# Strided sparse attention into a rational MLP on one core: an order drawn from plays with shared DMA queues and instruction lines, small matmuls in pieces, and the last 512 tokens in two chunks

## What is computed

```python
rel = pos[:, None] - pos[None, :]
mask_local = (rel >= 0) & (rel < 32)                                   # heads 0 to 3
mask_strided = (rel >= 0) & (pos[None, :] % 32 == pos[:, None] % 32)   # heads 4 to 7
attn = softmax(where(mask, q @ k.T / 8, -1e9)) @ v
x = attn.transpose(0, 2, 1, 3).reshape(4608, 512)
h = x @ w_in                                                           # 512 -> 2048
P = a[0] + a[1] * h + a[2] * h**2 + a[3] * h**3
Q = 1 + |b[0]| * |h| + |b[1]| * h**2
out = (P / (Q + 1e-6)) @ w_out                                         # 2048 -> 512
```

## Time and profile before

| | us |
|---|---|
| median of 3 runs | 437.22 |
| lowest, highest | 433.15, 437.31 |
| the profiled execution's own time | 436.66 |
| its span, first to last instruction | 434.8 |

### The profile page before, as it was taken

One profiled execution on the slowest core, in us unless ns is written; L12 is line 12 of the kernel. 1 busy time (PEld: TensorE's weight loads), 2 busy tenths in 40 slices (PEclk: granted clock), 3 DMA queues, 4 the chain that ended last, 5 costly groups with the idle time before them and its releaser, 6 DMA issues.

```text
span 434.8 us, 10010 instructions
## 1 busy us (share of the span) xinstructions
PE 339.6 (78%) x4494; PEld 170.3 (39%) x4540; DVE 322.3 (74%) x237; ACT 313.5 (72%) x332; POOL 110.0 (25%) x122
## 2 busy tenths in 40 slices
PE   1636975768997987488787989699899989958437
PEld 1426334434453443234433545254445434423212
DVE  5232198796989587568859879988989789897760
ACT  3211557296978796298749988888889999979732
POOL 6950391670009238063225320000000000000000
PEclk9999996696998999699969999699999999969959
DMA  9999999994559999999949994121121101101102
GB/s 192 173 205 134 163 174 141 150 170 65 115 154 88 148 172 178 148 144 174 129 116 126 175 115 105 24 54 73 30 51 51 50 1 48 50 0 48 48 0 96
DMA packets 140466, 46.52 MB, mean 107 GB/s; under 512 B 112376, under 2 KB 135160, under 8 KB 140280
## 3 DMA queue, kind: packets, MB, share of 16 engines
q0 software_dynamic: 77024, 17.19, 48.5%
q1 hardware_dynamic: 63112, 28.56, 35.9%
q10 hardware_dynamic: 288, 0.14, 0.1%
HBM read 36.87 MB, written 17.69 MB: 125 GB/s over the span
## 4 chain that ended last, share of the span: by engine, by line
PE 41%; ACT 26%; DVE 13%; DMA 11%; issue 8%; SPq 1%
PE ps L898 15%; PE ps L958 14%; ACT u L932 8%; ACT u L927 7%; ACT z L914 4%; ACT h L903 4%; PE ps L852 4%; DMA ptS<-pS 4%; DMA coef<-in_moe_b_dram 3%; DMA ptL<-pL 2%; PE ps L726 2%; DVE h L944 2%; DVE u L923 2%; DMA XT<-xl 2%; DVE z L941 2%
## 5 line engine op out<-in xcount | busy, mean ns | idle before, releaser
L958 PE MATMUL ps<-Wout,h 128*128 128x512 bf16 x557 | 142.3, 395 | 25.7 <-DVE h L944 19.8
L898 PE MATMUL ps<-XT,Win 128*128 128x512 bf16 x549 | 144.5, 398 | 12.3 <-issue 6.4
L903 ACT ACTIVATE h<-ps 128x512 bf16<-128x512 f32 x144 | 80.7, 620 | 38.1 <-PE ps L898 37.3
L958 PEld LDWEIGHTS ps<-Wout,h 128*128 128x128 bf16 x576 | 56.2, 101 | 95.4 <-DVE h L944 21.8
L898 PEld LDWEIGHTS ps<-XT,Win 128*128 128x128 bf16 x576 | 54.8, 102 | 78.6 <-issue 15.5
L927 ACT ACTIVATE u<-u,consts 128x2048 bf16<-128x2048 bf16 x36 | 70.4, 2005 | 3.7 <-DVE u L923 3.6
L932 ACT ACTIVATE u<-u 128x2048 bf16<-128x2048 bf16 x36 | 67.0, 1914 | 0.0
L914 ACT ACTIVATE z<-h 128x2048 bf16<-128x2048 bf16 x32 | 60.1, 1941 | 0.1
L476 POOL DMA_DIRECT2D lq<-in_q_dram x14 | 31.2, 2230 | 81.3 <-DMA skT<-sk 81.3
L944 DVE TENSOR_TENSOR h<-z,u 128x4096 bf16<-128x4096 bf16 x18 | 41.2, 2290 | 2.6 <-ACT u L932 2.2
L592 POOL DMA_DIRECT2D vN<-in_v_dram x32 | 37.9, 2283 | 18.3 <-PE ps L783 16.9
(11 more groups left out here) (76 smaller groups left out, 291.0 us busy)
## 6 DMA issues: line engine op xcount, KB each, us to landing
out_dram<-os SPq DMA_DIRECT2D x36, 256.0 KB, 2.4
vN<-in_v_dram POOLq DMA_DIRECT2D x32, 72.0 KB, 12.9
vS<-in_v_dram POOLq DMA_DIRECT2D x32, 72.0 KB, 10.8
Win<-in_moe_w_in_dram POOLq DMA_DIRECT2D x8, 256.0 KB, 15.0
Wout<-in_moe_w_out_dram POOLq DMA_DIRECT2D x4, 512.0 KB, 7.1
lq<-in_q_dram POOLq DMA_DIRECT2D x14, 144.0 KB, 6.6
lk<-in_k_dram POOLq DMA_DIRECT2D x14, 144.0 KB, 7.6
sq<-in_q_dram POOLq DMA_DIRECT2D x7, 288.0 KB, 9.2
```

The costliest lines, as they stand in the source:

```text
L898: r = e.matmul(bank(ph, 0, CH), Win[:, kk, f * 128:(f + 1) * 128], XT[:, kk, c * CH % XC:c * CH % XC + CH], start=(kk == 0), stop=(kk == N ...
L903: P.op("act", lambda e, f=f, ph=ph, h=h: e.activation(h.t[:, f % G, :], bank(ph, 0, CH), AF.Copy), 0.597, ky, r=[ph], w=[h], occ=0.494)
L958: r = e.matmul(bank(po, 0, Fout), groups[g].t[:, j, m * 128:(m + 1) * 128], Wout[:, kk, :], start=(kk == 0), stop=(kk == NF - 1))
```

## The change

The planner keeps its list scheduling (now `_draw`) and gains three things: a count of PE's instructions in lines of 256, with 3.5 us from the end of one line to the arrival of the one after the next; a second simulation, `_play`, that runs a finished order with two DMA queues which slow each other down; and a loop that draws an order, plays it, feeds the landing times of the play back (averaged with the earlier ones) and keeps the order with the shortest play of twelve. Each PE operation carries its number of instructions `ni` (8 unless given).

```diff
+LINE, FETCH = 256, 3.5
+DRAWS = 12
...
+    def _fetch(self, st, t, o, commit):
+        cnt, land = st[0], st[1]
+        step = o.dur / o.ni
+        left = o.ni
+        while left:
+            line, at = divmod(cnt, LINE)
+            if at == 0 and line >= 2:
+                t = max(t, land[line])
+            n = min(left, LINE - at)
+            t += n * step
+            cnt += n
+            left -= n
+            if cnt % LINE == 0:
+                nx = max(t, land.get(line + 1, 0.0)) + FETCH
...
+    def _draw(self, lag):
...
+                    if e == "pe" and o.ni > 20 and s <= t0 + 1e-9:
+                        late = self._fetch(line, s, o, False) - s - o.dur
+                        if late > 0.3:
+                            s += late
...
+                if lag is None:
...
+                else:
+                    o.fin = t + lag[o]
+            elif e == "pe":
+                o.fin = self._fetch(line, t, o, True)
+                free[e] = o.fin
...
+    def _play(self):
...
+        def rate(k):
+            if not (que[0] and que[1]):
+                return 1.0
+            return 0.38 if k else 0.46 if que[1][0].dma[2:] else 0.27
...
+    def schedule(self):
+        for o in self.ops:
+            o.deps0 = dict(o.deps)
+        lag, best = None, None
+        for n in range(DRAWS):
+            self._draw(lag)
...
+            span = self._play()
+            if best is None or span < best[0]:
+                best = (span, keep)
+            new = {o: o.fin - o.start for o in self.ops if o.dma is not None}
+            lag = new if lag is None else {o: 0.5 * (x + lag[o]) for o, x in new.items()}
```

```diff
-        def lscore(e):
+        def lscore(e, g):
             r = None
-            for g in range(3):
...
+        for g in range(3):
+            P.op("pe", lambda e, g=g: lscore(e, g), 16 * 0.012, key, r=[lqt, lkt], m=[SL], ni=32)
...
-        P.op("pe", sscore, 128 * 0.009, ky, r=[T_c, sqt, skt], m=[SS])
+        for i in range(4):
+            P.op("pe", lambda e, i=i: sscore(e, i), 32 * 0.0095, ky, r=[T_c, sqt, skt], m=[SS], ni=64)
...
-            P.op("pe", sav, 64 * 0.010, key, r=[ptS, vS], w=[A])
+            for j in range(2):
+                P.op("pe", lambda e, sav=sav, j=j: sav(e, j), 32 * 0.0145, key, r=[ptS, vS],
+                     ni=64, **(dict(m=[A]) if j else dict(w=[A])))
```

```diff
+    for src, t, T in ((q, sq0, T_s0[0]), (k, sk0, T_s0[1])):
+        for b4 in range(4):
+            P.op("sp", lambda e, src=src, t=t, b4=b4: e.dma_start(
+                view0(t, 72, 2048)[:, 512 * b4:512 * b4 + 512],
+                bass.AP(tensor=src.tensor, offset=src.offset + HL * S * D + 512 * b4, ap=[[2048, 72], [1, 512]])),
+                0.45, -15e5 + b4, w=[T[b4]], dma=(0.45, 1.9))
```

```diff
-    def mlp(c, key):
+    def mlp(t0, n, gf, key):
...
+        fb = 512 // n
+        W = gf * n
+        part = W / 4096
...
+                    for j in range(fb):
+                        for kk in range(NK1):
+                            r = e.matmul(bank(ph, j * n, n), Win[:, kk, (f + j) * 128:(f + j + 1) * 128],
+                                         XT[:, kk, t0 % XC:t0 % XC + n], start=(kk == 0), stop=(kk == NK1 - 1))
...
+    todo = [(CH * c, CH, G) for c in range(NT // CH - 1)]
+    at = NT - CH
+    for n, gf in [(256, 8), (256, 8)]:
+        todo.append((at, n, gf))
+        at += n
```

More of the change, by code:

```diff
@@ L96, in op @@
         o.pre = [d for d in dict.fromkeys(pre)]
+        o.ni = ni
         for t in r:
@@ L127, in _place @@
         return best
-    def schedule(self):
+    def _fetch(self, st, t, o, commit):
[12 more added lines that the diff above has]
+                nx = max(t, land.get(line + 1, 0.0)) + FETCH
+                if commit:
+                    land[line + 2] = nx
+                elif line + 2 not in land:
+                    land = dict(land)
+                    land[line + 2] = nx
+        if commit:
+            st[0] = cnt
+        return t
+    def _draw(self, lag):
         E = self.ENG
         for o in self.ops:
-            o.then = []
+            o.then, o.users = [], []
+            o.deps = dict(o.deps0)
+            for b in o.banks:
+                b.left = 0
         for o in self.ops:
@@ L147, in schedule @@
         dmafree = {}
+        line = [0, {0: 0.0, 1: 0.0}]
         for o in self.ops:
@@ L805, in attention @@
         t0 = b * S
-        war = []
-        for c in range(t0 // CH, (t0 + S - 1) // CH + 1):
-            war += up_of.get(c - XC // CH, [])
+        war = [o for x, n, ops in up_of if x + XC < t0 + S and t0 < x + n + XC for o in ops]
         for t in T_xl[b]:
@@ L921, in mlp, with pair @@
-            dv(lambda e, z=z, u=u: e.tensor_scalar(u.t[:, :, :], z.t[:, :, :], b1_ap, b0_ap, op0=Alu.mult, op1=Alu.add),
+                dur = 0.2 + (dur - 0.2) * part
+                return P.op("dve", fn, dur, ky + dk * part, occ=dur - 0.08, **kw)
+            def pair(fn, dur, dk, **kw):
+                half = W // 2
+                dur = 0.165 + (dur - 0.165) * part
+                return [P.op("act", lambda e, i=i: fn(e, slice(half * i, half * i + half)), dur, ky + dk * part, occ=dur - 0.1,
+                             **({k: [x[i]] if k == "after" else x for k, x in kw.items()})) for i in range(2)]
@@ L949, in mlp @@
+            dv(lambda e, zf=zf: e.tensor_scalar(zf, zf, a_ap[0], None, op0=Alu.add), 1.28, 13, m=[z])
+            dv(lambda e, zf=zf, uf=uf, hf=hf: e.tensor_tensor(hf, zf, uf, op=Alu.mult), 2.28, 14, r=[z, u], m=[h])
+            groups.append((h, hf.rearrange("p (g c) -> p g c", c=n)))
+        ky = key + 46 * n / 512
         ends = []
[L950 removed]
+        for m in range(n // 128):
             po = Banks(1)
[L952 to L964 removed]
@@ new lines, in mlp, with mm @@
+            for f0 in range(0, NF, 4):
+                h, hv = groups[f0 // gf]
+                def mm(e, m=m, f0=f0, po=po, hv=hv):
+                    r = None
+                    for kk in range(f0, f0 + 4):
+                        r = e.matmul(bank(po, 0, Fout), hv[:, kk % gf, m * 128:(m + 1) * 128], Wout[:, kk, :],
+                                     start=(kk == 0), stop=(kk == NF - 1))
+                    return r
+                kw = dict(m=[po]) if f0 else dict(w=[po])
+                if f0 == 0 and m >= OPEN:
+                    kw["after"] = ends[m - OPEN:m - OPEN + 1]
+                last = P.op("pe", mm, 0.864, ky + m * 7.6 + f0 * 0.475, r=[h, T_wout[f0 // 8]], **kw)
```

307 lines of the change are left out of this document (172 added, 135 removed).

## The result

| | before | after |
|---|---|---|
| median in the runs beside each other, us | 436.68 | 421.35 |
| lowest, highest | 433.15, 437.31 | 420.62, 423.06 |
| ratio, 95% interval | | 0.967 [0.961, 0.973] |
| the profiled execution, its span | 436.66, 434.8 | 421.98, 420.2 |

Faster by 3.3%; forecast were 418 us, from 402 to 435. The total came near, and the three terms behind it did not. I cut each profiled span at two instructions of VectorE (DVE) that every version has: the first operation of its first MLP group after the absolute value (L921, now L1079), and the same operation of the sixteenth group, the last that has 4096 columns after the change.

A forecast was written before the change was run, and what follows sets the result against it. No engine was taken as full; DVE and ACT wait for a stage in front, partly PE's instruction-fetch stalls. 436.7 - 11 (middle) - 2 (start) - 6 (tail) = 417.7, so 418 us, range 402 to 435.

The forecast's parts named there:

- The tail, forecast -6: Last 512 tokens as two chunks of 256: shorter final matmuls -5.5, DVE waits -2.2, added operations +1.3 and +0.6 us.
- half should go: -2.2: Tail: DVE's waits of 2.20 and 2.21 us for ACT halve, as the pair of ACT passes is half as long.
- the 1.3 forecast: Tail: cost of 16 more DVE operations at 80 ns each, 1.3 us, within 0 to 3.5.
- ACT's 0.6 us: Tail: cost of 12 more ACT passes, taken as 0.6 us within 0 to 2.3.
- The middle, forecast -11: From 60 to 270 us: line planning removes most of PE's 14.9 us of stalls before small attention matmuls, 11 us gained.
- The reading of the stalls as line ends: PE stalls before small attention matmuls come when a line of some 256 instructions ends before the next is fetched; 14.9 us.
- the second rival: Fetch stalls move to the next boundary without shrinking; only start and tail gain, 429 us; chance 0.23.
- I take 0 beyond the fetch term: Middle: truer DMA landing times and the redrawn order bring 0 us besides fewer fetch stalls; bounds 22 us either way.
- The start, forecast -2: Start: loads in quarters and sqT copies set before the coef operation gain 2 us, within 1.3 to 3.4, or 0.
- The coef wait: Start: DVE waits 3.35 us for coef before copying sqT; the planner can set the copy first.
- Banks: Rival: waiting pieces hold PSUM banks, so up-projections wait for ACT's copies; 28 to 30 us lost, 446 us; chance 0.15.
- The order gaining more: Rival: the better drawn order speeds 60 to 270 us by 22, with start -3 and tail -6: 406 us; chance 0.17.

The follow-up runs named there:

- e1: The changed kernel with its last 512 tokens as one chunk of 512 again; 430.2 us, ratio 0.983 to the kernel before.
- e6: The kernel before with only the last 512 tokens split into two chunks of 256; 425.9 us, ratio 0.978 to the kernel before.
- e2: The changed kernel with the planner's fetch time set from 3.5 us to 0, pieces and plays kept; 422.0 us, ratio 0.965 to the kernel before.
- e4: The changed kernel with the start of before (two whole loads, transposes and copies by column block); 411.7 us, ratio 0.941 to the kernel before.
- e7: The changed kernel, same planned order, its eight start copies writing two neighbouring elements one after the other; 416.1 us, ratio 0.950 to the kernel before.
- e12: e7 with the planner also told, as in e9, that a q or k load holds SP 2.8 us; 416.7 us, ratio 0.956 to the kernel before.
- e11: e7 with the spacing of the chunks' keys at 33.1 for 33.0, altering only the order drawn; 421.4 us, ratio 0.968 to the kernel before.
- e13: e4 with the planner also told, as in e9, that a load holds SP 2.8 us; 411.6 us, ratio 0.942 to the kernel before.
- e9: The changed kernel with the planner told that each transposing q or k load holds SP 2.8 us, not 1.25; 420.2 us, ratio 0.964 to the kernel before.

## Why the forecast was right in its sum and wrong in its terms

**The tail, forecast -6, measured -9.2 (at its place 9.9 in e1 and 9.3 in e6).** The mechanism held, and one term was mis-sized. The drain after the last DVE operation went from 14.4 us (420.35 to 434.8) to 8.6 (411.57 to 420.2), -5.8 for -5.5; its matmuls, of which 15 are recorded, began at the lower level of the clock and were in the right range, against 11.24 us in the earlier trace rows. PE alone (busy, granted clock, DMA share, GB/s):

```profile
411.60:414.40 2.80, 2.60 (x6) 0.54 0.00 0
414.40:417.00 2.60, 2.50 (x9) 0.84 0.00 0
```

The step that failed is "half should go: -2.2". On DVE the stretch fell from 49.1 to 45.7 us, -3.4 where -2.2 + 1.3 were forecast. The waits for ACT there, 0.67 + 2.20 + 2.21 = 5.1 us before, are down to the 0.66 at 403.30. Four half groups give the planner two to interleave, so one runs where the other waits: two of them take 15.2 us together (387.43 to 402.63), 7.6 each, while the last, alone, takes 8.27 (403.30 to 411.57); half of a full group's 14.7 would be 7.34. So all of the waits but 0.66 went, -4.4, and the smaller operations cost 45.7 - 0.66 - 3 x 14.7 = 1.0 us for the 1.3 forecast. ACT's 0.6 us were not seen on the path.

**The middle, forecast -11, measured -5.7 (good to some 5 us).** The reading of the stalls as line ends held: the trace shows them again at regular distances, 0.9 to 4.2 us long. Two steps failed. First, "the planner now counts instructions in lines of 256 ... and postpones a piece that would stall". Counted in matmul and load records the longer stalls come some 253 apart, but some matmul records are missing: after's trace has all 4604 weight loads and only 4548 of as many matmuls. Second, that what PE waits is what the time loses: of 7.2 us of stalls gone, some came back as the wait for ptS, and e2 has 5.2 us more of them and the same time. That the model does not shorten the program was the second rival's core ("each saved stall is paid at the next boundary"), although the stalls did fall. "I take 0 beyond the fetch term" failed too: from e6 to e4, which adds line model, plays, pieces and the planner's new durations to the tail with the start of before, the time falls by 14 us. The first three were taken back only with the new start, where it does not show, and the durations never.

The sentence of the Trainium skill that the prediction weighed ("Runtime: NRT & Kernel Launch", "Instruction fetch mechanics": crossing a block is mostly hidden) would have left hardly a stall before or after; the 8 us stall of e2 speaks against that where small matmuls run in a row. For what the line model is worth to the time, nothing that e2 can tell, its 0 was nevertheless nearer than my 11.

**The start, forecast -2, measured +0.4 at the first group.** The coef wait of the earlier trace rows did go: the copies of sqT come first. The step that failed is the price of the edit as SP issues and PE waits alone: the changed copies were not priced at all. Eight copies at 1.4 to 1.6 us for 0.48 cost 3.7 and 4.9 us at the first group (e7, e12), more than the 1.3 to 3.4 us that were to be won. With the copies mended the quarters do bring what was forecast: the first group starts at 51.28, 51.45 and 51.91 us in e7, e11 and e12, and at 54.02 and 53.17 in e4 and e13, which have the old start. That e4 is 9.6 us faster all the same comes from the order drawn with the old start, in the middle; that the quarters as such cost it is not shown.

**The rivals.** Banks: PE's waits at L1053 (was L898) for ACT's copies of `h` are 0.6 us, so it did not come. The order gaining more is where e4 comes nearer, at 411.7 for its 406. So 418 came out near 421.35 by luck in part: the tail gave 3 us more than forecast, and a start that lost and a middle that gave half took away 7.7.

Of what was to show it: the drain is under 8 us, 6.0 from DVE's end (411.57) to the end of the last copy (417.58, row below), and the order of the copies is as said; the small stalls, at 7.7 us, miss the 6; DVE is at 83.6% from 60 to 330 us, just over the 83.

```profile
416.98 0.60 ACT L1112 ACTIVATE os<-ps 128x512 f32<-128x512 f32 x1 [0.27 <-PE ps L1103]
```

## What to carry to other kernels

Price an edit by every instruction whose access pattern it alters, also when the counts and sizes stay the same, and look at those rows first when a start gets no shorter. A stall on an engine that is not the bottleneck is not a sum to be collected: take it away alone (here e2 and e9) before calling it time. Cutting the last group in two pays twice, once in the drain after the last element operation and once because two halves fill each other's waits. Where an order is drawn anew by every edit, run the same order twice before reading a difference of some us out of it.

## What the runs showed of the hardware that was not expected

- A copy from PSUM of 128x288 to bf16 that writes 2-byte elements 16 bytes apart took 1.43 to 1.61 us, on DVE and ACT alike; with elements 4 bytes apart 0.48 to 0.49, with neighbouring pairs 0.42 to 0.46.
- PE's "issue" stalls of over 0.7 us in front of small matmuls, all but one, stand 256 of its instructions apart, or multiples of that, when loads, matmuls and the recorded semaphore instructions are counted; in all fourteen traces the first of them is at 451. They are up to 8.0 us long.
- Four transposing DMAs in a row held SP for 2.3 to 3.8 us each (231.81 to 243.39 us of after), so the one that stood behind three of them started 9 us after its data was there. Around 175 us such a DMA held SP for 1.3 to 1.6 us.
